# Attention, routed experts and MLP on one core: r and k arrive already turned, the attention products are cut into halves of TensorE's array, and GpSimd scales r

## The reference

```
for t in range(S):                     # attention, per batch and head
    cur = outer(u * k[t], v[t])
    y[t] = r[t] @ (state + cur)        # state is 48 x 48
    state = w[:, None] * state + outer(k[t], v[t])
...
logits = x @ w_gate                    # x: (2, 768, 384), eight experts
e = argmax(logits) or the expert of the token before, by a local gate
out = softmax(logits)[e] * (relu(x @ w1[e]) @ w2[e])
...
x + relu(layernorm(x) * g_ln @ w_ch1) @ w_ch2
```

## Time and profile before

| | |
|---|---|
| time, median of 3 runs (lowest to highest) | 433.4 us (433.09 to 434.15) |
| span of the profiled execution | 428.4 us |
| TensorE busy over the span | 392.5 us |
| VectorE, ScalarE, GpSimd busy | 233.5, 139.4, 127.5 us |

### The profile page before, as it was taken

One profiled execution on the slowest core, in us unless ns is written; L12 is line 12 of the kernel. 1 busy time (PEld: TensorE's weight loads), 2 busy tenths in 40 slices (PEclk: granted clock), 3 DMA queues, 4 the chain that ended last, 5 costly groups with the idle time before them and its releaser, 6 DMA issues.

```text
span 428.4 us, 7294 instructions
## 1 busy us (share of the span) xinstructions
PE 392.5 (92%) x2640; PEld 372.0 (87%) x2640; DVE 233.5 (54%) x440; ACT 139.4 (33%) x283; POOL 127.5 (30%) x128
## 2 busy tenths in 40 slices
PE   6799999995049999999999999899999999999993
PEld 5799999894049999999999999788998899988993
DVE  6887879974406573663745769586303652133110
ACT  0424536320007254372553735452002220022000
POOL 4685653613705235053250521300100001100010
PEclk9999999955559999999999999999999999999998
DMA  7998984063534869577584270410010001000000
GB/s 114 154 248 209 249 213 73 20 227 124 203 116 148 256 228 364 178 271 261 201 314 159 102 261 1 128 59 2 18 38 18 0 2 37 27 13 2 18 20 37
DMA packets 62250, 54.77 MB, mean 128 GB/s; under 512 B 41216, under 2 KB 56960, under 8 KB 62208
## 3 DMA queue, kind: packets, MB, share of 16 engines
q1 hardware_dynamic: 47744, 19.58, 18.8%
q10 hardware_dynamic: 12032, 26.74, 18.1%
q0 software_dynamic: 2432, 7.92, 4.8%
HBM read 43.13 MB, written 11.10 MB: 127 GB/s over the span
## 4 chain that ended last, share of the span: by engine, by line
PE 82%; DVE 6%; issue 4%; DMA 3%; ACT 2%; SPq 1%; POOL 0%; DVEq 0%; ACTq 0%; POOLq 0%
PE bank L1200 21%; PE bank L1202 21%; PE bank L1201 21%; PE bank L1162 4%; PE bank L1159 3%; PE bank L1147 3%; PE bank L1137 2%; PE bank L1171 2%; PE bank L1113 2%; PE bank L1195 1%; DMA kn<-in_k 1%; PE bank L1126 1%; DVE split L365 1%; PE bank L1212 1%; DMA xrow<-xsort 1%
## 5 line engine op out<-in xcount | busy, mean ns | idle before, releaser
L360 ACT CAST split<-raw 128x1024 fp32r<-128x1024 f32 (+1 forms) x60 | 59.2, 1004 | 0.0
L1200 PE MATMUL bank<-xT,split 128*128 128x256 f32 x192 | 55.1, 287 | 2.1 <-DVE xT L901 2.1
L1202 PE MATMUL bank<-xT,split 128*128 128x256 f32 x192 | 54.8, 286 | 0.0
L1201 PE MATMUL bank<-xT,split 128*128 128x256 f32 x192 | 54.8, 286 | 0.0
L365 DVE TENSOR_TENSOR split<-raw,split 128x1024 fp32r<-128x1024 f32 (+1 forms) x40 | 52.9, 1337 | 1.8 <-ACT split L360 1.7
L590 POOL DMA_INDIRECT out<-orow,cpos x12 | 11.6, 970 | 133.4 <-DVE orow L1030 133.4
L1200 PE MATMUL bank<-split,h2T 128*128 128x384 f32 x144 | 48.7, 338 | 0.0
L1202 PE MATMUL bank<-split,h2T 128*128 128x384 f32 x144 | 48.2, 335 | 0.0
L1201 PE MATMUL bank<-split,h2T 128*128 128x384 f32 x144 | 48.1, 334 | 0.0
L365 POOL TENSOR_TENSOR split<-raw,split 128x1024 fp32r<-128x1024 f32 (+1 forms) x20 | 45.8, 2305 | 5.7 <-ACT split L360 3.4
L1042 DVE SCALAR_TENSOR_TENSOR h2T<-bank,h2T 128x512 fp32r<-128x512 f32 x36 | 24.9, 691 | 38.0 <-ACT h2T L702 37.8
(11 more groups left out here) (166 smaller groups left out, 764.3 us busy)
## 6 DMA issues: line engine op xcount, KB each, us to landing
raw<-in_w ACTq DMA_DIRECT2D x14, 1536.0 KB, 7.3
raw<-in_w_ch ACTq DMA_DIRECT2D x2, 2304.0 KB, 9.0
xsort<-zeros SPq DMA_DIRECT2D x8, 388.0 KB
X<-xsort SPq DMA_DIRECT2D x8, 388.0 KB, 5.8
ysort<-yrow POOLq DMA_DIRECT2D x8, 388.0 KB, 7.0
raw<-in_w SPq DMA_DIRECT2D x2, 1536.0 KB, 8.2
X<-ysort SPq DMA_DIRECT2D x3, 776.0 KB, 6.2
rn<-in_r SPq DMA_DIRECT2D x12, 192.0 KB, 4.8
```

Source lines behind the costliest of these rows:

```text
L360: act.copy(hi, src).then_inc(s_hi, 1)
L1200: pe.matmul(dst, stationary[0], moving[0], start=first, stop=False)
L1201: pe.matmul(dst, stationary[0], moving[1], start=False, stop=False)
L1202: return pe.matmul(dst, stationary[1], moving[0], start=False, stop=last)
```

## The change

The host now lays out what the core loads. r and k arrive twice: turned, in one array `rkT` of 128 partitions by 1024 values per chunk, and as rows (`rows_kr`, 768 values per partition). v comes as rows of 384, and the experts' weights, the MLP's and the router's in contiguous pieces per partition. The eight transposes of r and k per chunk are gone. GpSimd multiplies r by its decay table (`rT`), ahead of `rk` and `ks`; VectorE multiplies k (`kT`), now from SBUF instead of PSUM. The state is kept as 48 columns per head. Its update is eight products of 128 rows by 64 columns of the array, the part of y from the state eight products of 64 rows by 128 columns, and the eight products from the scores follow these. y lies in two banks, which VectorE adds to X in two instructions. `rk`, `rku` and `ks` have 384 values per partition instead of 512, the state 192 instead of 384. v has four buffers instead of three.

```diff
@@ SyncE: loads
-                sp.dma_start(rn[q][:, :, 0:Dh], r[b, :, rows, :].rearrange("h t d -> t h d")).then_inc(s_r[q], 16)
-                sp.dma_start(kn[q][:, :, 0:Dh], k[b, :, rows, :].rearrange("h t d -> t h d")).then_inc(s_k[q], 16)
+                sp.dma_start(tin[q][:], rkT[i]).then_inc(s_t[q], 16)
...
+                sp.dma_start(kr[q][:], rows_kr[i]).then_inc(s_kr[q], 16)
@@ GpSimd
-                    pool.wait_ge(s_r[i % RING], 16 * (i // RING + 1))
-                    pool.wait_ge(s_k[i % RING], 16 * (i // RING + 1))
-                    pool.tensor_tensor(rk[b][:], rn[i % RING][:], kn[i % RING][:], ALU.mult).then_inc(s_rk, 1)
+                    if i == 0:
+                        pool.wait_ge(s_tab, 1)
+                    pool.wait_ge(s_t[i % RING], 16 * (i // RING + 1))
+                    need(pool, s_yp, i - 2)
+                    pool.tensor_tensor(rT[i % 3][:], tin[i % RING][:, 0], wp, ALU.mult).then_inc(s_rT, 1)
+
+                    need(pool, s_rku, i - B + 1)
+                    pool.wait_ge(s_kr[i % RING], 16 * (i // RING + 1))
+                    pool.tensor_tensor(rk[b][:], kr[i % RING][:, 1].rearrange("p h d -> p (h d)"),
+                                       kr[i % RING][:, 0].rearrange("p h d -> p (h d)"), ALU.mult).then_inc(s_rk, 1)
@@ VectorE
-                    dve.wait_ge(s_rkt, i + 1)
+                    dve.wait_ge(s_t[i % RING], 16 * (i // RING + 1))
 
                     need(dve, s_scp, i - B + 1)
-                    need(dve, s_yp, i - 2)
-                    dve.tensor_tensor(rT[i % 3][:], bank[0][:].rearrange("p (n t) -> p n t", n=NP), wp, ALU.mult).then_inc(s_rT, 1)
-                    dve.tensor_tensor(kT[b][:], bank[1][:].rearrange("p (n t) -> p n t", n=NP), wn, ALU.mult).then_inc(s_kT, 1)
+                    dve.tensor_tensor(kT[b][:], tin[i % RING][:, 1], wn, ALU.mult).then_inc(s_kT, 1)
...
-                    dve.tensor_tensor(X[:, j, 0:D], bank[4][:, 0:D], dv[b][:].rearrange("p h d -> p (h d)"),
-                                      ALU.add).then_inc(s_x, 1)
+                    for h in range(2):
+                        last = dve.tensor_tensor(X[:, j, 0:D].rearrange("p (n a d) -> p n a d", n=NP, a=2)[:, :, h],
+                                                 bank[h][:, 0:NP * Dh].rearrange("p (n d) -> p n d", n=NP),
+                                                 dv[b][:].rearrange("p (n a) d -> p n a d", a=2)[:, :, h], ALU.add)
+                    last.then_inc(s_x, 1)
@@ TensorE
-                    for src, bk in ((rn[i % RING], 0), (kn[i % RING], 1)):
-                        for n in range(NP):
-                            last = pe.transpose(bank[bk][:, n * P:(n + 1) * P],
-                                                src[:, 2 * n:2 * n + 2, :].rearrange("p h d -> p (h d)"), ident[:])
-                    last.then_inc(s_rkt, 1)
...
                     for n in range(NP):
-                        last = pe.matmul(bank[5][:, n * 2 * Dh:(n + 1) * 2 * Dh], ks[b][:, n, :],
-                                         vn[j % RING][:, 2 * n:2 * n + 2, :].rearrange("p h d -> p (h d)"), start=True, stop=True)
+                        for h in range(2):
+                            q = slice(h * HALF, (h + 1) * HALF)
+                            last = pe.matmul(bank[5][q, n * Dh:(n + 1) * Dh], ks[b][:, n, q], vn[j % VRING][:, 2 * n + h, :],
+                                             start=True, stop=True)
...
+                            pe.matmul(bank[h][:, n * Dh:(n + 1) * Dh], rT[j % 3][q, n, :], state[b][q, n, :],
+                                      start=(n == 0), stop=False)
```

More of the change, by code:

```diff
@@ L32, with program @@
 GATE_EDGE = -1.5 * 2.0 ** -23
[L35 to L39, removed]
+def program(nc, rkT, rows_kr, rows_v, w, u, w_small, wexp, wch, gain_in, out, xsort, ysort, dims):
+    B, H, S, Dh, E, F, F2 = dims
+    D = H * Dh
     CH = S // P
@@ L50, in program @@
     RING = 3
+    VRING = 4
     WT = 2
@@ L63, in program @@
     NPH = len(PHASES)
-    assert D == H * Dh and H * HALF == 512 and KF == 8 and D <= 384
+    assert H * HALF == 512 and KF == 8 and D <= 384
     ctx = ExitStack()
@@ L167, in program @@
         winv = attn("winv", [P, 2, NP])
-        ub, _ = at("rows", 9216, "ub", [P, H, HALF])
+        ub, _ = at("rows", 9216, "ub", [P, H * Dh])
         wp = attn("wp", [P, NP, P])[:, :, :]
@@ L171, in program @@
         wnT = attn("wnT", [P, NP * P])[:, :]
[L172 to L175, removed]
+        wst = attn("wst", [P, NP, Dh])
+        tin = [at("rows", 13312 + 4096 * i, f"tin{i}", [P, 2, NP, P])[0] for i in range(RING)]
+        kr = [attn(f"kr{i}", [P, 2, H, Dh]) for i in range(RING)]
+        vn = [attn(f"vn{i}", [P, H, Dh]) for i in range(VRING)]
         rT = [attn(f"rT{i}", [P, NP, P]) for i in range(3)]
         kT = [attn(f"kT{b}", [P, NP, P]) for b in range(B)]
-        rk = [attn(f"rk{b}", [P, H, HALF]) for b in range(B)]
-        rku, _ = at("rows", 11264, "rku", [P, H, HALF])
+        rk = [attn(f"rk{b}", [P, H * Dh]) for b in range(B)]
+        rku, _ = at("rows", 11264, "rku", [P, H * Dh])
         ks = [attn(f"ks{b}", [P, NP, P]) for b in range(B)]
         sc = [attn(f"sc{b}", [P, 2, NP, P]) for b in range(B)]
-        state = [attn(f"state{b}", [P, NP, 2 * Dh]) for b in range(B)]
-        stsum = [attn(f"stsum{b}", [P, NP, 2 * Dh]) for b in range(B)]
+        state = [attn(f"state{b}", [P, NP, Dh]) for b in range(B)]
+        stsum = [attn(f"stsum{b}", [P, NP, Dh]) for b in range(B)]
         dg = [sb(f"dg{b}", [P, H]) for b in range(B)]
@@ L212, in program @@
         xnT = split[0][:, :, CN:WN].rearrange("p z (q t) -> p z q t", q=KD)
-        s_r = [sem(f"r_in{b}") for b in range(RING)]
-        s_k = [sem(f"k_in{b}") for b in range(RING)]
-        s_v = [sem(f"v_in{b}") for b in range(RING)]
+        s_t = [sem(f"rkT_in{b}") for b in range(RING)]
+        s_kr = [sem(f"kr_rows_in{b}") for b in range(RING)]
+        s_v = [sem(f"v_in{b}") for b in range(VRING)]
         s_blank = sem("blank_zeroed")
@@ L737, in _ @@
             link(dve.tensor_tensor(wsq[:, 1 - a, :], wsq[:, a, :], wsq[:, a, :], ALU.mult))
[L738 to L741 removed]
+            dve.tensor_copy(wst[:], wsq[:, 1 - a, :].unsqueeze(2).broadcast_to([P, NP, Dh]))
             link(dve.tensor_copy(wn, wp[:, :, ::-1]))
@@ L1158, in _ @@
                     for n in range(NP):
-                        pe.matmul(bank[4][:, n * 2 * Dh:(n + 1) * 2 * Dh], rT[j % 3][:, n, :], state[b][:, n, :],
-                                  start=True, stop=False)
                         for h in range(2):
-                            last = pe.matmul(bank[4][:, (2 * n + h) * Dh:(2 * n + h + 1) * Dh], sc[b][:, h, n, :],
-                                             vn[j % RING][:, 2 * n + h, :], start=False, stop=(h == 1))
+                            q = slice(h * HALF, (h + 1) * HALF)
+                            pe.matmul(bank[h][:, n * Dh:(n + 1) * Dh], rT[j % 3][q, n, :], state[b][q, n, :],
+                                      start=(n == 0), stop=False)
+                    pe.wait_ge(s_sc, 2 * (j + 1))
+                    pe.wait_ge(s_v[j % VRING], 16 * (j // VRING + 1))
+                    for n in range(NP):
+                        for h in range(2):
+                            last = pe.matmul(bank[h][:, n * Dh:(n + 1) * Dh], sc[b][:, h, n, :], vn[j % VRING][:, 2 * n + h, :],
+                                             start=False, stop=(n == NP - 1))
                     last.then_inc(s_yp, 1)
@@ L1321 @@
         args.append(nc.dram_tensor(f"in_{name}", a.shape, F32, kind="ExternalInput").ap())
-    B, H, S, Dh = r.shape
-    rows, D = B * S, H * Dh
     out = nc.dram_tensor("out", (rows, D), F32, kind="ExternalOutput").ap()
-    xsort = nc.dram_tensor("xsort", (moe_w_gate.shape[1] * (rows + 2 * P), D + 4), F32, kind="Internal").ap()
+    xsort = nc.dram_tensor("xsort", (E * (rows + 2 * P), D + 4), F32, kind="Internal").ap()
     ysort = nc.dram_tensor("ysort", (rows + 2 * P, D + 4), F32, kind="Internal").ap()
-    program(nc, *args, out, xsort, ysort)
+    program(nc, *args, out, xsort, ysort, (B, H, S, Dh, E, F, F2))
     got = run_bass_kernel_spmd(nc, [arrays], core_ids=[0])
```

113 lines of the change are left out of this document (54 added, 59 removed).

## The result

The changed kernel takes **460.8 us** (median of 4 runs, 456.8 to 464.5) against 433.7 us of the kernel before (4 runs, 433.1 to 434.2): a ratio of 1.061, 95% interval 1.057 to 1.065. The profiled execution has a span of 455.1 us (before 428.4), which is 26.7 us more. Its run took 456.8 us, so only 1.7 us lie around a span. By that figure the profiled execution of before took 430.1 us, 3.6 less than the median, and the 5.0 us of the prediction mixed the two.

The account below looks back on a forecast made before the run. TensorE's own work was taken as the bound nearly everywhere. First update at 12.2 and mostly 11.0 us half-clock passes end the stage at 138.7, 39.3 later: 428.4 + 39.3 = 467.7, plus 5.0 around it, 473 us; range 432 to 486.

Parts of the forecast that it names:

- The decision in the start-up: Before the first state update, TensorE idles and the clock falls to half at about 12 us, or a pass later.
- survives the start: Rival: the clock stays full through the start-up and the stage gains; 429 us, or 423 with the cheapest update; chance 0.12.
- The clock stays at 0.50: Attention stage: once fallen, the clock stays at half until the experts' dense products; chance 0.60, 473 us.
- The half-clock pass: One pass of TensorE in the attention stage at half clock: 11.0 us.
- The update: State update, 16 instructions on half the columns, priced like the scores: 1.91 us at half clock, 1.10 at full.
- The wait ahead of X's transposes: Behind the logits in each pass at full clock, TensorE waits 0.2 us for VectorE's X.
- The stage's end: End of the attention stage at 138.7 us, 39.3 later than before.
- The start: Start-up: tables ready at 8.2 us, wn's transposes from 8.3 to 9.0, first state update at 12.2.
- GpSimd and VectorE at no cost: Attention stage: the multiplications moved to GpSimd and VectorE cost nothing, hidden by TensorE's pass; without cover up to 0.5 us a pass.
- The rival of new waits: Clock kept, but VectorE's two-input operations wait behind GpSimd's twice a pass, taking the passes' gain away: 433 us; chance 0.05.
- At full clock: One pass of the attention stage at full clock takes 6.3 us, 0.35 less than 6.66.
- Behind the stage: Routing, scatter, experts and MLP follow the attention stage in an unchanged chain and keep their lengths.

Follow-up runs that it names:

- run 1: Changed kernel with y's 16 products per chunk moving 96 columns instead of 48, in the same number of instructions: 425.1 us, ratio 0.982.
- run 4: Changed kernel with eight unread transposes of the identity per chunk where those of r and k stood: 432.4 us, ratio 0.996.
- run 5: Changed kernel with its layout and GpSimd's rT, but state, update and y in pairs as before: 432.3 to 454.6 us, median 448.9.
- run 12: Changed kernel with only the y-state products moving 96 columns, the y-scores products keeping 48: 440.5 us, ratio 1.016.
- run 2: Changed kernel with the start-up filled by 34 more blank products in the first burst and 54 behind wn's transposes: 457.8 us, ratio 1.054.
- run 7: Kernel of run 1 with the logits in a bank of their own: 425.6 us, ratio 0.984.
- run 6: Kernel of run 1 with the multiplication of r by its decay table back on VectorE: 424.9, 430.1, 424.9 and 430.2 us.
- run 11: Kernel of run 7 with blank products: 14 ahead of pass 11's logits, 8 ahead of pass 12's X, 34 ahead of er's transposes: 422.1 us, ratio 0.978.
- run 8: Kernel of run 7 with 200 blank products behind the last router product, in the gap before the experts: 440.0 us, ratio 1.019.

## Why the prediction came out as it did

The forecast was 473 us, slower; it is slower, 460.8 us, and the cause forecast (half clock in the attention stage, without the work that the change takes away) is what runs 1, 4, 5 and 12 show. Part of the agreement is luck: the forecast hung on the start-up, which decides nothing, and the same step would have given 429 us had the clock survived there. By its own steps:

- **The decision in the start-up** ("Start-up, where I expect the decision") is the step that failed. The clock did fall there, at 8.6 rather than 12 us (at 11.5 in run 1), but run 2 took that fall away and the median changed by 3 us, and run 1 left it there and got the clock back at 21.7. What decides is what a pass of the loop does. The rival "survives the start" was priced at 429 us on the assumption that a clock that survives also holds; run 2 is that case, and it takes 457.8. The right row stood in the prediction all the same: 15.34 busy of 15.50 us at 0.50 from 83.80 to 99.30.
- **"The clock stays at 0.50"** holds for most of the stage, not for all. It came back four times, 16.6 us in all. By the two passes measured, 10.62 and 5.98 us, those 16.6 us did what takes 29.5 at half clock: 12.9 us of the miss, an estimate and an upper one, since TensorE idled in 2.13 us of the first such stretch (15.50 to 22.20).
- **The half-clock pass**, 11.0 forecast, is 10.62. The update was the mis-sized term: its 16 instructions take 1.03 us at half clock and 0.60 at full, near the lower bound (0.95 and 0.45), not the scores' price (1.91 and 1.10). Each takes 0.038 us at full clock against 0.113 for a full-array one. Two that run side by side wholly would take 0.057 each, so each is also shorter by itself, as its weight load is (0.137 us against 0.191, run 1). How much each of the two gives is not shown. The scores (1.87 for 1.91), y-state (1.71 for 1.67) and y-scores (3.45 for 3.58) were right. Page "TensorEngine Tiling (Array Packing)" of the Trainium skill (Key Properties) has tiles loading and multiplying in parallel; the update's 0.038 us is in line with it.
- **The wait ahead of X's transposes** was forecast as 0.2 us for VectorE's X. In the middle passes it is 0.35 us for ScalarE's copy of the logits, which shares their bank; VectorE's X is done by then. I had looked for who writes the operand, not for who still reads the bank. Before, the eight transposes hid it; run 7 removes it.
- **The stage's end** was forecast at 138.7 and came at 125.39. The 12.9 us at full clock and 8 x 0.38 us of shorter passes would make it 16.0 us earlier; it is 13.3, so 2.7 us went the other way. The second update's wait of 1.75 us for the state sum in the start-up is part of that, and the upper estimate of 12.9 another; the rest was not followed up.
- **The start:** first update at 12.2, seen 12.07; tables ready at 8.2, seen 8.24; wn's transposes as forecast. `rT` 1.82 instead of 1.32, with `kT` beside it from 8.25 to 8.94: the sum had `kT`'s 0.68 and `rT`'s 1.32 one behind the other, to 10.2, and `rT` ended at 10.06.
- **GpSimd and VectorE at no cost:** right. `rT` takes 1.55 us on average and `kT` 1.07, both longer than their alone times, and TensorE waits for neither in the loop. Run 6 moves `rT` back and does not gain. The rival of new waits falls.
- **At full clock** the passes would be 5.98 us (forecast 6.3). The rival "the clock survives" had 423 us with the cheap update; run 1, the nearest to it (y's products wider, full clock from 21.7 us), took 425.1.
- **Behind the stage** nothing changed: from its end to the experts' first product 25.9 us; before it was 25.8, from 99.39 to 125.22.

Page "TensorE: Matmul & The Clock Gate" of the Trainium skill (Part 1) says that steady work brings 2.4 GHz back. The trace does not agree: 55.71 busy of 57.80 us at 1.2 GHz, and 65.98 of 68.10 in run 2. The same page (Part 4) says that work in TensorE's transpose mode does not count as busy for the clock in the same way. The profile lists the transposes here as MATMUL and does not name a mode; if they are in that mode, run 4 does not agree either: eight idle transposes per chunk took the changed kernel from 460.8 to 432.4 us. What exactly the chip weighs is not settled by these runs; shown is that added work on TensorE, by transposes or by more columns in the same instructions, raises the share of the stage at full clock.

## What to carry to other kernels

Work removed from TensorE in a stage of small fp32 products can cost more than it saves: read the granted clock of each stretch beside the busy share, because TensorE can be busy 96% of the time at half clock. Where an instruction costs the same whatever it moves, let it move more: the doubled columns of run 1 cost no time to be seen and turned 6% slower into 2% faster. And when a wait is taken away from one engine, ask who still reads the bank that the next instruction writes, and put fillers in the very wait where the clock is lost (run 11), and not ahead of an engine's own work that the gap had hidden, as the register loads of run 8 seem to have been.

## What the runs showed of the hardware that was not expected

- In one unchanged loop the granted clock comes and goes without a gap in TensorE's work: run 4 was busy 16.80 of 16.80 us at 1.00 around a stretch of 3.20 of 3.20 at 0.50. It comes and goes in runs 5 and 12 too, with some gaps. The spread from run to run is then wide, 432.3 to 454.6 us in run 5, where run 1's four lie within 0.4 us.
- At full clock 16 instructions on column halves of the array (the update) take 0.60 us, 16 on row halves (y-state) 0.96, 16 on the full array 1.86 (run 1). The column halves take a third of the full array's time, the row halves half.
- Behind a filling of blanks, TensorE was given one or two instructions every 1.4 us for 7 us while GpSimd's indirect transfers ran, one every 1.27 us (run 8), though the first 47 blanks had passed beside the same transfers. Work put into that gap was not free, and what followed it was delayed.
